# Moving the split of a fetched bilinear unit behind the third ReLU, an index read ahead of a wait, and one low part into the last attention batch

## The reference, cut to what matters

```
scores = scale * q @ k.T;  ret = scores * decay(i - j >= 0);  x = ret @ v          # per head, causal, (2304, 512)
e_idx = argmax(x @ w_gate);  gate_w = softmax(x @ w_gate)[e_idx];  eom = sigmoid(x @ w_output_gate)
for e in range(8):                                                                # top-1 experts
    h = relu(x[mask] @ w1[e]);  y[mask] = gate_w * eom[:, e] * (h @ w2[e])
out = ((y @ w_a) * (y @ w_b)) @ w_out                                             # bilinear layer
```

## Time and profile before

| | us |
|---|---|
| median of 3 runs | 777.29 |
| lowest and highest run | 774.27 and 777.62 |
| the profiled execution's own time | 774.47 |
| its span in the profile | 772.6 |
| TensorE busy in the span | 756.5 (98%) |
| VectorE, ScalarE, GpSimd busy | 481.9, 281.4, 79.1 |

### The profile page before, as it was taken

One profiled execution on the slowest core, in us unless ns is written; L12 is line 12 of the kernel. 1 busy time (PEld: TensorE's weight loads), 2 busy tenths in 40 slices (PEclk: granted clock), 3 DMA queues, 4 the chain that ended last, 5 costly groups with the idle time before them and its releaser, 6 DMA issues.

```text
span 772.6 us, 14934 instructions
## 1 busy us (share of the span) xinstructions
PE 756.5 (98%) x5488; PEld 697.8 (90%) x5490; DVE 481.9 (62%) x906; ACT 281.4 (36%) x500; POOL 79.1 (10%) x110
## 2 busy tenths in 40 slices
PE   8999998999999999999999999999999999999996
PEld 6887867999999999999899999999999999999994
DVE  5578777677667676656666787447553555544371
ACT  4555643555455564532132332212321221221121
POOL 2000022101101101100011100301110030111003
PEclk9999999999999999999999999999999999999998
DMA  9989836497788789588832667875453566444402
GB/s 170 231 222 253 225 112 202 134 360 242 263 317 291 238 304 315 183 312 305 327 124 82 247 252 304 299 275 213 139 202 143 201 253 237 161 180 163 177 1 82
DMA packets 116598, 168.82 MB, mean 219 GB/s; under 512 B 63948, under 2 KB 83439, under 8 KB 116527
## 3 DMA queue, kind: packets, MB, share of 16 engines
q1 hardware_dynamic: 112205, 156.93, 59.6%
q0 software_dynamic: 4176, 10.92, 4.4%
q10 hardware_dynamic: 146, 0.04, 0.0%
HBM read 131.34 MB, written 36.54 MB: 217 GB/s over the span
## 4 chain that ended last, share of the span: by engine, by line
PE 76%; SPq 10%; DMA 6%; issue 3%; DVE 2%; POOL 0%; DVEq 0%; ACT 0%; POOLq 0%
PE pz L2075 34%; PE po L2100 19%; PE py L2020 9%; PE pu L2009 6%; DMA bilinear_weights<-w_lo 5%; SPq L573 4%; SPq L630 2%; PE pu L1991 1%; PE pout L1813 1%; PE pscore L1759 1%; SPq L569 1%; PE pq L1773 1%; PE px L1962 1%; SPq L654 1%; PE pu L1999 1%
## 5 line engine op out<-in xcount | busy, mean ns | idle before, releaser
L2075 PE MATMUL pz<-x_hi,w_hi 128*128 128x384 f32 x504 | 171.0, 339 | 0.4 <-DVE u L1618 0.3
L2075 PE MATMUL pz<-x_hi,w_lo 128*128 128x384 f32 x504 | 170.1, 338 | 0.0
L2075 PE MATMUL pz<-x_lo,w_hi 128*128 128x384 f32 x504 | 169.8, 337 | 0.0
L1618 DVE TENSOR_TENSOR u<-pz,p 128x384 f32<-128x384 f32 x72 | 40.1, 557 | 116.0 <-PE pz L2075 115.9
L2075 PEld LDWEIGHTS pz<-x_hi,w_hi 128*128 128x128 f32 x504 | 94.7, 188 | 4.9 <-DVE a_sb L1618 1.0
L2075 PEld LDWEIGHTS pz<-x_lo,w_hi 128*128 128x128 f32 x504 | 94.9, 188 | 0.7
L1082 ACT COPY p<-pz 128x384 f32<-128x384 f32 x36 | 17.3, 480 | 213.7 <-PE pz L2075 213.7
L2075 PEld LDWEIGHTS pz<-x_hi,w_lo 128*128 128x128 f32 x504 | 94.8, 188 | 0.0
L2100 PE MATMUL po<-wo_hi,g_hi 128*128 128x512 f32 x216 | 84.3, 390 | 0.0
L2100 PE MATMUL po<-wo_hi,g_lo 128*128 128x512 f32 x216 | 84.3, 390 | 0.0
L2100 PE MATMUL po<-wo_lo,g_hi 128*128 128x512 f32 x216 | 84.2, 390 | 0.0
(11 more groups left out here) (262 smaller groups left out, 1301.5 us busy)
## 6 DMA issues: line engine op xcount, KB each, us to landing
land<-in_moe_w_dram SPq DMA_DIRECT2D x64, 512.0 KB, 8.1
w_hi<-bilinear_weights SPq DMA_DIRECT2D x31, 896.0 KB, 4.5
w_lo<-bilinear_weights SPq DMA_DIRECT2D x31, 896.0 KB, 6.4
bilinear_weights<-w_hi SPq DMA_DIRECT2D x12, 896.0 KB, 11.6
bilinear_weights<-w_lo SPq DMA_DIRECT2D x12, 896.0 KB, 12.2
wo_land<-in_moe_w_out_dram SPq DMA_DIRECT2D x18, 512.0 KB, 3.7
q_in<-in_q_dram SPq DMA_DIRECT2D x32, 128.0 KB, 3.3
k_in<-in_k_dram SPq DMA_DIRECT2D x32, 128.0 KB, 3.2
```

Of the source, the lines that this page charges most:

```text
L1618: nc.vector.tensor_tensor(dst, pz[n % 2][:, 0:T], more, ALU.add).then_inc(z_kept_dve, 1)
L2075: ins = nc.tensor.matmul(pz[n % 2][:, 0:T], w, m, start=(k in FRESH and j == 0 and i == 0), stop=(j == DH2 - 1 and i == 2), skip_group_che ...
```

## The change

1. In every expert after the first, ScalarE and VectorE handle the fetched unit later: `stage_high(.., 0)`, `stage_combine` and `stage_low(.., 0)` move from ahead of block 0 to behind block 2; `stage_high(.., 1)` goes behind `relu(3)`, `stage_low(.., 1)` behind `rest(4)`. The last window is changed alike.
2. SyncE reads the next expert's number before it waits for `began`, not after.
3. VectorE's low part of unit 3 moves from behind the window table (just after `starts_ready`) into the last attention batch, at tile 3, ahead of that tile's `keep_logits`.
4. TensorE's 13 products without use become ten float32r products of 224 and 112 columns in turn on `w_hi[0]`, with a wait for `hi_done` that has long been met, and 7 of the old kind.

```diff
@@ sync
                 if first:
+                    expert = sp.value_load(order[0:1, e + 1:e + 2], min_val=0, max_val=E - 1)
                     sp.wait_ge(began, b + 1)
                     sp.sem_inc(alone_sp, 1)
-                    expert = sp.value_load(order[0:1, e + 1:e + 2], min_val=0, max_val=E - 1)
@@ scalar, body
-                if first and e > 0:
-                    stage_high(e - 1, 0)
                 for f in range(NPU):
                     relu(f)
                 if first and e > 0:
+                    stage_high(e - 1, 0)
+                relu(NPU)
+                if first and e > 0:
                     stage_high(e - 1, 1)
-                for f in range(NPU, NPU + 2):
-                    relu(f)
+                relu(NPU + 1)
@@ vector, last batch
+                    if last and c == TOGETHER:
+                        first_low(*first_units(b, c - 1, first, last))
                     if c >= 1 and not (last and c > TOGETHER):
                         keep_logits(b, c - 1)
@@ vector, behind starts_ready
-            first_low(3, 5)
@@ vector, body
+                for f in range(NPU):
+                    rest(f)
                 if first and e > 0:
                     stage_combine(e - 1)
                     stage_low(e - 1, 0)
-                for f in range(NPU):
+                for f in range(NPU, NPU + 2):
                     rest(f)
                 if first and e > 0:
                     stage_low(e - 1, 1)
-                for f in range(NPU, 5):
-                    rest(f)
@@ tensor
-            wait_busy(13)
+            pe.wait_ge(hi_done, 1)
+            for n in (STEP * R, R) * 5:
+                nc.tensor.matmul(pscore[1][:].rearrange("p j t -> p (j t)")[:, 0:n], w_hi[0][:, 0, 0:P], w_hi[0][:, 0, 0:n],
+                                 start=True, stop=True)
+            wait_busy(7)
```

More of the change, by code:

```diff
@@ L1055, in last_body @@
                 w = WIDTH[E - 1]
-                stage_high(E - 2, 0)
                 for f in range(FF):
-                    if f == NPU:
-                        stage_high(E - 2, 1)
+                    if NPU <= f < NPU + 2:
+                        stage_high(E - 2, f - NPU)
                     act.wait_ge(up_done, b * FF + (f + 1))
@@ L1588, in rest @@
                                                    op0=ALU.max, op1=ALU.subtract).then_inc(h_lo_ready, 1)
-                stage_combine(E - 2)
-                stage_low(E - 2, 0)
                 for f in range(FF):
                     if f == NPU:
+                        stage_combine(E - 2)
+                        stage_low(E - 2, 0)
+                    if f == NPU + 2:
                         stage_low(E - 2, 1)
```

## The result

The changed kernel took 772.15 us in the median of 20 executions (771.36 to 774.27), the kernel before 776.28 us (773.42 to 782.15, 20 executions). The ratio is **0.9944, 95% interval 0.9927 to 0.9961**: 4.1 us faster. The forecast was 776.5, and 0.89 of its chances stood on a change of less than 0.5%.

The account below looks back on a forecast made before the run. TensorE, busy 98% of the span, bounds the kernel. Its path could give 2.0 + 0.1 us, SyncE's chain 0.65 + 0.1; the smaller, 0.75, off the median 777.29 gave 776.5, range 773.2 to 778.6.

Parts of the forecast that it names:

- Part 1, inside the experts: Experts, lines 1999 to 2009: no wait for `h_lo` remains, nothing new is late (slack 0.5 us or more), cost nothing.
- late second low part: SyncE's store of the fetched unit: the low part ends about 6 us behind line 1999, formerly 3; later issue free.
- Part 1, what it removes: Third, fifth and last experts: losses of 1.2, 0.3 and 0.5 us, together 2.0 us on TensorE's path, all removed.
- What takes the place of the wait: Start of the bilinear layer: TensorE arrives 2.0 us earlier, finds unit 0 not there; SyncE's chain decides the gain.
- (a): TensorE's path: all 2.1 us stay, unit 0's data landing 1.3 us earlier than worked out; 775.2, chance 0.17.
- (c): TensorE around 110 to 125 us: slower runs lose clock, which the ten products can keep up; 773.5, chance 0.11.
- (d): TensorE at 114 to 121 us: thinner work lowers the clock for the first expert's start; 779.5, chance 0.06.
- (b): SyncE's rings swallow the index read and the wait at 350.77 only grows: no gain; 777.3, chance 0.12.
- (e): Last window: the later second low part delays unit 6's store, slower where TensorE isn't ahead; 778.3, chance 0.04.
- Part 2, 0.65 us: Second expert: reading the index before the wait starts SyncE's chain, and lands unit 0, 0.65 us earlier; bounds 0 and 0.75.
- Part 3, 0.1 us: Last attention batch: moved low part costs nothing, may speed GpSimd's third gather issue; gain 0 to 0.2, taken 0.1.
- Part 4, 0: TensorE before the third gathered block: exchanged idle products change its time by -0.6 to +1.7 us; taken as 0.

Follow-up runs that it names:

- all but the split: Whole change without the later handling of the fetched unit (index read, low part and products only), against the kernel before: 777.85 us, 1.0022.
- first series: Whole change against the kernel before, 20 executions each: 772.15 us, 0.9944; its profiled execution took 771.57 us.
- second series: Whole change timed again on another chip, 12 executions, against the kernel before: 776.15 us, 1.0000.
- parts 1 and 2 alone: Only the later handling of the fetched unit and the earlier index read, against the kernel before: 774.70 us, 0.9979.
- With unit 0 freed: Only the later split, with unit 6 neither stored nor waited for and unit 5's copy read instead, against the kernel before: 772.97 us, 0.9953.
- the same omission: Kernel before with unit 6 neither stored nor waited for and unit 5's copy read instead, against the kernel before: 775.77 us, 0.9997.
- the change with the swap: Whole change with unit 6's store issued ahead of unit 1's fetch, against the kernel before, two series: 772.46 us, 0.9958; 771.68 us, 0.9945.
- The split alone: Only the later handling of the fetched unit, behind the third ReLU, against the kernel before: 777.69 us, 1.0013.

## Why the prediction was wrong, point by point

**Part 1, inside the experts: right.** No wait for `h_lo` is left in any of the four profiles of the change, nothing new is late there, and the third expert's turn is 1.68 us where 1.57 were worked out. The late second low part cost nothing either: the store of unit 6 went out at 328.65.

**Part 1, what it removes: the mechanism right, the size wrong.** In the profile it was 1.8 us, not 2.0. The undisturbed turn was taken as 1.66 us from a row of the chain; read like the others, from timelines, the sixth expert's is 266.68 - 264.93 = 1.75, and the fifth expert's group of 11 was one of 12 whose start, 236.69, lay ahead of the stretch in the earlier trace rows. More important, this was the loss of one execution, and a good one. Other profiled executions without the split wait 2.3 us (index read alone), 3.4 (all but the split), 3.8 (low part alone) and 7.9 (products alone) for `h_lo`, where the earlier trace rows have 1.4, and three of the seven profiled kernels without the split pay 1.7 or 3.4 us of clock on top, in the third expert. The prediction put the profile's difference on the median. The profile lay 2.8 us under that median, and the profiles say that the slower executions are slower mostly by the very waits that the change removes and the clock behind them. For the executions without a profile there is only the mean granted clock, listed with each time except for the kernel before in the first series; it goes the same way. One fall of 1.7 us in some 772 is 0.002 of the mean:

| mean clock of the execution | before: executions, median | whole change: executions, median |
|---|---|---|
| 0.997 and more | 76 of 160, 774.75 | 39 of 56, 772.2 |
| 0.995 and 0.996 | 60 of 160, 777.45 | 12 of 56, 773.6 |
| 0.994 and less | 24 of 160, 779.34 | 5 of 56, 778.3 |

In the first row the change gains 2.5 us, about what part 1 was costed at before the forecast let unit 0's fetch take most of it back; the rest goes with fewer executions in the two lower rows (30% instead of 52%). Why a lower mean clock goes with up to 4.6 us more, of which the clock itself makes only a part, is not told by this table; in the profiles four of the seven falls come behind long waits.

**"What takes the place of the wait": this step failed.** It said that unit 0's fetch moves by SyncE's 0.65 us alone, to 343.4, since no edit makes a transfer shorter, and that TensorE would wait 1.2 to 1.5 us for it. It was issued at 339.55 in the first profile and there was no wait. (By the prediction's own terms the wait would have been 0.29 + 2.0 - 0.65 = 1.6 us, a little over the 1.2 to 1.5 it gave.) The error was to take a chain of transfers for a chain of fixed length. The traces show that the time from a store's issue to its landing moves with what was issued ahead of it and when. At 300.04 in the kernel before, the store's issue took 3.88 us, behind the next expert's weights, and the raw fetch followed 16.3 us later; in the change it was held 0.94 us, and 13.15 us passed (311.79 - 298.64). In the last window the store of unit 6 was issued only 0.92 us earlier, but unit 1 had been fetched 4.6 us earlier: it used the time from 326 to 328 us, in which the DMAs of the kernel before moved next to nothing. So less stood ahead of the store, and it landed 10.5 us after its issue instead of 14.0. At 338 to 341 us, when the kernel before still moved 432 GB/s, the change moves 33. Stretches 326 to 328 us of the kernel before and of the change, the landing of unit 6's low part (KB, median us from issue to landing) in the same order, and the stretch 338 to 341 us of the change:

```profile
326.00:328.00 2.00, 2.00 (x15) 2.00 (x14) 1.37 (x2) 0.79 (x2) 0.00 (x0) 1.00 0.21 40
326.00:328.00 2.00, 2.00 (x15) 2.00 (x15) 1.68 (x4) 0.79 (x2) 0.00 (x0) 1.00 1.07 395
...
bilinear_weights<-w_lo SPq DMA_DIRECT2D x1, 896.0 KB, 14.0
bilinear_weights<-w_lo SPq DMA_DIRECT2D x1, 896.0 KB, 10.5
...
338.00:341.00 3.00, 3.00 (x23) 2.99 (x22) 1.85 (x4) 2.01 (x4) 0.00 (x0) 1.00 0.17 33
```

**As a description the step was half right.** In some executions the read-back is what TensorE waits for: 1.3 us in the second series' profile, just the size forecast, 1.3 again without the low part, 1.6 without the products, 4.5 plus the clock with parts 1 and 2 alone. So the forecast described one case among several and took it for the only one. In the second series' profile the whole working fits: unit 0 fetched at 343.12 (343.4 forecast), the first `pz` product at 349.85 (350.0), the execution's own time 773.53 (773.7). With unit 0 freed the split gave 0.9953, and the same omission without the split 0.9997.

**The rivals.** What came is (a), all 2.1 us stay (775.2), plus an effect like (c), the clock in the runs (773.5), together. (c) had one part of it, that some of the 3 us between executions are the clock at its lower level: of the 32.7 us that waits for `h_lo` and the clock cost the seven profiled kernels without the split, the clock made 8.5. But it put part 4 down as what prevents it. The 20 profiled executions, both kernels and the eighteen experiments, were read from 60 to 760 us, up to 360 us in stretches of some 30 us; seven have a stretch with a mean clock under 0.97. Four stand behind a wait named above: three behind `h_lo`, in kernels without the split, and the one behind `w_lo`. Three are at the first expert, where (c) and (d) had looked: in the kernel before with unit 6 not stored, in the change without the low part, and in the change with the swap, whose stretches are

```profile
118.00:120.00 2.00, 0.96 (x7) 0.43 (x5) 1.76 (x12) 0.00 (x0) 0.00 (x0) 1.00 0.28 98
120.00:122.00 2.00, 1.54 (x9) 1.17 (x10) 1.19 (x4) 1.29 (x4) 0.00 (x0) 0.92 0.00 0
122.00:124.00 2.00, 2.00 (x9) 2.00 (x8) 2.00 (x5) 0.18 (x1) 1.05 (x2) 0.50 0.40 127
124.00:126.00 2.00, 2.00 (x11) 2.00 (x11) 1.20 (x2) 0.00 (x0) 1.70 (x2) 0.73 1.01 377
```

Two of these three have the ten products and one hasn't, of 11 and 9 profiled kernels with and without them. So the fall at the first expert is real, costs (0.08 + 0.50 + 0.27) x 2 = 1.7 us here, and nothing here says that the products hold it off. (b) and (e) didn't come.

**Part 2, 0.65 us:** SyncE's first load in the second expert starts at 151.65, before 153.20; 1.55 us earlier, of which the earlier start of TensorE explains about 1.0, so 0.5 to 0.6 for the read. Alone it gave 0.9979 (0.9955 to 1.0003), and the whole change without it 0.9963 (0.9940 to 0.9987). Its worth isn't resolved.

**Part 3, 0.1 us:** the third gather's issue took 0.93 us instead of 1.13, as estimated, and the runs can't tell it from nothing (0.9996 (0.9971 to 1.0022)). **Part 4, 0:** the ten products took 1.30 us, between the bounds 0.8 and 3.1 and nearer the lower one (the upper end, +1.7 us, would have been more than the 1.57 us in which TensorE stands and not 0.1 less, as the prediction has it); TensorE still waited 1.24 us for the third gather behind them. Alone 1.0020 (0.9994 to 1.0046): no effect is shown.

**Open.** Why one series of four gave 1.0000 with the same instructions. A late ring explains how such executions come about, and profiles show it, but why the second series had 5 of its 12 executions above 777 us and the three others none isn't known. Nor is it settled whether parts 2 to 4 add anything to the split. The split alone at 1.0013 and the whole at 1.0000 were measured on different chips from the good series, so that "the split needs the others" and "those chips are poor ones" can't be told apart; against the second stands that on the chip of the 1.0000 two kernels with one part less gave 0.9961 and 0.9963. And that unit 0's fetch is what made the split alone no gain is argued from profiles of other kernels; the split's own profile waits 0.3 us for it.

## What to carry to other kernels

A wait that shows 1 us in one profile may be 1 to 4 us over the executions. If the times of the runs lie 3 us apart and the profile shows the fastest, look for a race between two chains close to each other; an edit that lets one chain pass the point at which it waits for the other can be worth more in the median than in that profile. Add to a wait of TensorE of 1.8 us or more that the clock may fall behind it (here 1.7 to 3.4 us behind four of seven waits of 1.8 us and more), and don't move the end of a DMA chain by the shift of its first issue alone: look at what is issued ahead of each store, and how long ahead.

## What the runs showed that I had not expected

- **The clock behind a wait.** TensorE waited 1.84, 3.53 and 3.83 us in the third expert of three kernels, and the clock stood at 0.50 (1.2 GHz of 2.4) in stretches behind it, costing 1.7, 1.7 and 3.4 us; 1.7 again behind the 4.5 us wait at 350. Behind waits of 1.05, 1.99 (two profiles) and 2.78 us it stayed at 1.00. The length of the wait alone doesn't decide it.
- **The way from store to fetch.** With the same bytes, the fetch behind unit 6's store was issued 7.4 us after it (swap), 10.9 (first profile), 13.95 (second series) and 14.5 us (before), according to how long before the store 1.8 MB of another fetch had been issued.
- **Narrow products.** At full clock, ten products, alternately of 224 and 112 columns, took 1.30 us together, 0.13 each and 0.8 ns a column, against 0.46 ns a column at 304 columns.
